# Who issues the weight loads: all of them moved from SyncE's queue to GpSimd's own

## What is computed

```python
x = attention(q, k, v)        # 4 images, 8 heads, 576 positions, head size 64;
                              # mask: block of 64 queries sees its own and earlier blocks of 64 keys
x = transpose(x) -> (2304, 512)
h = x @ moe_w_in              # (512, 1024)
solu = h * softmax(h)
ln = (solu - mean) / sqrt(var + 1e-6) * g_ln
x = ln @ moe_w_out            # (1024, 512)
h = x @ moe2_w_in             # (512, 2048)
g = h * tanh(softplus(h))     # Mish
out = g @ moe2_w_out          # (2048, 512)
```

## Time and profile before

| | us |
|---|---|
| median of 3 runs | 710.01 |
| lowest, highest | 707.37, 711.13 |
| the profiled execution | 708.7 |
| its span | 706.7 |
| PE busy | 691.3 |
| DVE busy | 391.8 |
| ACT busy | 385.0 |
| POOL busy | 82.5 |

### The profile page before, as it was taken

The page is one execution under the profiler, slowest core; times in us unless marked ns, Lnnn a source line. Parts: engine busy times, 40 slices in busy tenths (PEclk is TensorE's granted clock), DMA queues, the critical chain, the costliest instruction groups (busy, mean ns, idle before and its releaser), DMA issues.

```text
span 706.7 us, 15716 instructions
## 1 busy us (share of the span) xinstructions
PE 691.3 (98%) x6490; PEld 465.0 (66%) x6490; DVE 391.8 (55%) x865; ACT 385.0 (54%) x824; POOL 82.5 (12%) x109
## 2 busy tenths in 40 slices
PE   8889999979999999999999999999999999999998
PEld 8558864558547864776468646784588457855873
DVE  6898787773575438543743586627543663352120
ACT  5677875456575555365555664646465554452230
POOL 3121027331000000320000000320000000000000
PEclk9999999999999999999999999999999999999999
DMA  9589875943066506531353176521524164023000
GB/s 273 116 199 212 239 190 134 201 94 58 27 120 127 109 9 117 100 94 45 65 80 77 30 139 130 124 72 29 114 46 61 22 134 91 3 39 74 17 16 30
DMA packets 158518, 68.12 MB, mean 96 GB/s; under 512 B 144368, under 2 KB 147952, under 8 KB 158448
## 3 DMA queue, kind: packets, MB, share of 16 engines
q1 hardware_dynamic: 158448, 67.13, 44.2%
HBM read 26.74 MB, written 4.72 MB: 45 GB/s over the span
## 4 chain that ended last, share of the span: by engine, by line
PE 81%; DVE 7%; ACT 5%; DMA 4%; issue 2%; SPq 0%; ACTq 0%; DVEq 0%
PE banks L805 24%; PE banks L824 24%; PE banks L787 12%; PE banks L774 11%; PE banks L753 4%; PE banks L726 4%; DMA pT<-halves 2%; DVE halves L903 2%; PE banks L715 1%; ACT prob L1054 1%; ACT WH L1078 1%; DVE nmax L890 1%; ACT halves L1062 1%; DMA q_raw<-q 1%; DMA lnT<-ln_split 1%
## 5 line engine op out<-in xcount | busy, mean ns | idle before, releaser
L805 PE MATMUL banks<-x2T_hi,WH 128*128 128x256 f16 x576 | 157.8, 274 | 0.5 <-DVE x2T_lo L974 0.4
L805 PE MATMUL banks<-x2T_lo,WH 128*128 128x256 f16 x576 | 157.8, 274 | 0.0
L805 PE MATMUL banks<-x2T_hi,WL 128*128 128x256 f16 x576 | 157.7, 274 | 0.0
L1054 ACT ACTIVATE prob<-banks,nmax 128x64 f32<-128x64 f32 (+8 forms) x144 | 74.9, 523 | 75.4 <-DVE nmax L890 44.9
L824 PE MATMUL banks<-WH,gT_hi 128*128 128x512 f16 x288 | 109.4, 380 | 0.0
L824 PE MATMUL banks<-WH,gT_lo 128*128 128x512 f16 x288 | 109.2, 379 | 0.0
L824 PE MATMUL banks<-WL,gT_hi 128*128 128x512 f16 x288 | 109.2, 379 | 0.0
L903 DVE SCALAR_TENSOR_TENSOR halves<-prob,rinv,halves 128x64 f16<-128x64 f32 (+8 forms) x144 | 86.7, 616 | 38.3 <-ACT halves L1062 38.1
L983 DVE SCALAR_TENSOR_TENSOR gT_lo<-gbuf,gT_hi 128x512 f16<-128x512 f32 x72 | 50.1, 706 | 101.6 <-ACT gT_hi L1134 101.2
L1062 ACT ACTIVATE halves<-prob,rinv 128x64 f16<-128x64 f32 (+8 forms) x144 | 75.7, 554 | 51.0 <-DVE rinv L898 32.8
L787 PE MATMUL banks<-lnT,WH 128*128 128x256 f16 x576 | 95.9, 273 | 0.0
(11 more groups left out here) (94 smaller groups left out, 997.2 us busy)
## 6 DMA issues: line engine op xcount, KB each, us to landing
w_raw<-w SPq DMA_DIRECT2D x12, 512.0 KB, 5.2
out<-osb SPq DMA_DIRECT2D x18, 256.0 KB, 2.8
q_raw<-q SPq DMA_DIRECT2D x16, 256.0 KB, 3.6
k_raw<-k SPq DMA_DIRECT2D x12, 288.0 KB, 3.5
ln_raw<-w SPq DMA_DIRECT2D x6, 512.0 KB, 4.1
v_raw<-va SPq DMA_DIRECT2D x12, 256.0 KB, 2.7
own_raw<-w SPq DMA_DIRECT2D x4, 512.0 KB, 5.4
pT<-halves SPq DMA_TRANSPOSE x80, 3.7
```

Of the source, the lines that this page charges most:

```text
L805: mm = pe.matmul(banks[:, MI_BANK[n % 2], G * j:G * (j + 1)], w2i(b, c, m), (x2T_hi, x2T_lo)[a][:, c], start=(c == 0 and i == 0), stop=(c ...
L1054: act.activation(prob[:, at:at + width(blk)], scores[:, at:at + width(blk)], ACT.Exp, bias=nmax[:, u % 2, i:i + 1], scale=1.0, accum_out=r ...
```

## The change

All 24 weight loads move from SP's program to POOL's, with the waits ahead of them. POOL issues the first five right after it has built the identity, and the other 19 at their places in `PLAN`. Loads of q, k, v and g_ln, the transposes and the stores stay on SP, in the same order. The amounts, the buffers and the semaphores that count the landings stay as they are.

```diff
@@ block.sync
             def load_w(piece):
                 room, n = room_of(piece)
-                if n > 1:
-                    wait_split(sp, ROOMS[room][n - 2])
-                elif 4 <= room < 6:
-                    sp.wait_ge(ln_lo, TPG)
-                elif 6 <= room < 8:
-                    sp.wait_ge(x2_done, 2)
                 sp.dma_start(raw_of(piece), w[piece]).then_inc(w_in[room], 16)
...
             load_q(0)
             load_first(k_first_raw, k, 1, k_first_in)
             load_first(v_first_raw, va, 0, v_first_in)
-            load_w(0)
             load_first(v_first_raw, va, 1, v_first_in)
-            load_w(1)
             load_q(1)
-            load_w(2)
-            load_w(3)
             sp.dma_start(gsc[:], g_ln).then_inc(g_in, 16)
-            load_w(4)
             load_k(0)
...
-                if kind == "load_w" and of[0] >= 5:
-                    load_w(*of)
@@ block.gpsimd
+            def load_later(piece):
+                room, n = room_of(piece)
+                if n > 1:
+                    wait_split(pool, ROOMS[room][n - 2])
+                elif 4 <= room < 6:
+                    pool.wait_ge(ln_lo, TPG)
+                elif 6 <= room < 8:
+                    pool.wait_ge(x2_done, 2)
+                pool.dma_start(raw_of(piece), w[piece]).then_inc(w_in[room], 16)
...
                                pattern=[[-1, P]], channel_multiplier=1).then_inc(const_pool, 1)
+            for piece in range(5):
+                load_later(piece)
             pool.wait_ge(const_pool, 2)
             pool.wait_ge(const_dve, 1)
             for kind, *of in PLAN:
...
                 if kind == "w2_split":
                     w2_split(*of)
+                if kind == "load_w" and of[0] >= 5:
+                    load_later(*of)
```

## The result

The changed kernel takes 730.7 us (median of 4 runs, 727.53 to 733.62), the kernel before on the same chip 709.92 (4 runs, 707.37 to 711.13). The ratio is 1.030, interval 1.027 to 1.034: **21 us slower**, where 7.6 were forecast. The profiled execution took 727.53 us. In it line 753 of before is L754 (values), 726 is L727 (scores), 824 is L825, 833 is L834; POOL's lines are 13 lower (3 in the splits of 20 to 23).

The account below looks back on a forecast made before the run. TensorE, busy 98% of the span, was taken as the bound; terms 1.3 + 0.6 + 4.0 + 1.7 = 7.6 us on the profiled 708.7 gave 716.3, forecast as 717.6 us for the median, range 712.0 to 724.6.

Parts of the forecast that it names:

- Place 3: Last three loads, 101 to 110 us: two landings lie bare on GpSimd between its splits, TensorE stalls 2L - 4.0, +4.0 us.
- L: Time from issue to landing of a weight load on GpSimd's queue, taken as 4.0 us, bounds 3.6 and 5.9.
- The clock: After TensorE's 4.0 us standstill at the last pieces, matmuls run partly at half clock: +1.7 us, bounds 0 and 1.7.
- Place 1: The start: one more weight served ahead of the second query tile delays TensorE, +1.3 us, bounds 0 and 3.8.
- the first keys and queries leave before it: At the start: first keys and queries leave before GpSimd's first weight load, so one more weight ahead, +1.3 us.
- Place 2: 58 to 60 us: weights 8 and 9 no longer stand behind the transpose of lnT, +0.6 us, bounds 0 and 2.5.
- Other moved issues cost nothing: Weights 5 to 19: each issue costs GpSimd some 0.5 to 1 us, covered by its other work; no term in the sum.
- Weights crowd out the start: Rival: all five weights served before the second query tile, +3.8, both loads hurt lnT, +2.5; 722.0 us, chance 0.18.
- Slow queue: Rival: transfers from GpSimd take over 6 us, stall above 8 us; 721.6 us and more, chance 0.05.
- Short landing: Rival: L is 3.0 us, stall 2.0, no clock loss, no cost at the start or lnT; 712.0 us, chance 0.12.
- Faster: Rival: SyncE's queue, freed of weights, removes TensorE's 4.3 us of idle time before 60 us; 705.7 us, chance 0.05.

Follow-up runs that it names:

- the probe run: Kernel before plus seven dead loads of weight piece 0 from 210 us on, issued by GpSimd, SyncE or ScalarE, all weights on SyncE; one execution, 708.7 us.
- e: Kernel before with pieces 0 to 4 on GpSimd, piece 0 gated on the second keys, 1 to 4 on the second query tile; 710.95 us, ratio 1.0033.
- d: Kernel before with pieces 0 to 4 issued by ScalarE ahead of its table load, all others by SyncE; 712.87 us, ratio 1.0059.
- a: Kernel before with only pieces 0 to 4 issued by GpSimd, the other 19 by SyncE; 713.26 us, ratio 1.0044.
- f: Kernel before with pieces 5 to 19 on GpSimd, load 7 placed later and loads 10 to 12 moved back in the plan; 714.46 us, ratio 1.0089.
- c: Kernel before with only pieces 20 to 23 issued by GpSimd; median 716.0 us, ratio 1.0092.

## Why the prediction was wrong

**Place 3, the last pieces: right in mechanism, near in size, partly by luck.** Forecast a stall of 2L - 4.0 = 4.0 us with L = 4.0. Loads 20 to 23 landed in 3.8, 4.3, 4.8 and 5.4 us; the lag of PE rose by 4.1 us from 108.7 to 121.99, of which the wait for piece 23 is 2.9 and one for a transpose 1.0. Split 20 ended 15.3 us later than before, at 118.75 us, and 118.0 + 4.3 + 4.8 + 15.3 = 142.4 is the end of split 23 to 0.2 us (the memset's 0.3 hides under load 22's landing; without it 142.1). PE was 17.3 us late by then, 2 us more than POOL, so the stall came out 2.9 and not 5.1: landings longer than forecast and a later PE partly cancelled, and the 1.0 us for a transpose, which was not in the sum, brought the rise back to the forecast 4. The sentence that delays of places 1 and 2 carry both engines along and therefore add was only nearly right; with the last four alone, PE was 3.4 us late for another reason and the stall was 0.3 us. By the Trainium skill (DMA: Bandwidth & Descriptors, Anatomy of one DMA), L would have been 3.2 us, an estimate; the trace has 3.8 to 5.4.

**The clock: right as a kind of cost, wrong in place and count.** No loss behind place 3: the granted clock from 142.3 to 146.3 us is 1.00. It fell elsewhere, behind waits that were not forecast (1.9 us before 19.52, 1.9 before 61.07 and 4.7 before 86.49 us). The windows of after that show it:

```profile
19.50:26.50 7.00, 6.98 (x62) 6.03 (x62) 6.43 (x16) 2.90 (x10) 2.25 (x2) 0.76 0.24 56
60.00:66.00 6.00, 4.93 (x61) 4.28 (x62) 5.43 (x11) 3.67 (x8) 1.02 (x1) 0.72 0.38 70
84.00:88.00 4.00, 1.51 (x24) 1.15 (x28) 0.00 (x0) 0.94 (x3) 2.98 (x5) 0.75 0.71 127
```

Length times one less the clock gives 1.7, 1.7 and 1.0 us; 0.7 more follow from 88 to 92 us (clock 0.83). That is 5.1 us, and PE is busy 5.8 us longer, against a forecast of 1.7. Not every such loss is the change's: the probe run, the same as the kernel before up to 210 us, has one from 29 to 34 us, where the kernel before has 1.00 behind the same wait of 1.70 us:

```profile
29.00:34.00 5.00, 4.09 (x31) 1.63 (x32) 4.04 (x14) 3.55 (x13) 0.00 (x0) 0.66 0.53 101
```

So one loss of 1.7 us more or less is scatter between executions, and which of the changed kernel's losses each wait brought is not shown. That they are more is: the mean granted clock of its four executions is 0.986 to 0.991, that of the 29 executions of the kernel before beside the last group 0.993 to 1.00, 0.998 in the mean. Over the span that is 8.6 us lost (0.0118 x 729) against 1.6, so some 7 of the 21 us are the clock's.

**Place 1, the start: term 1.3, bounds 0 and 3.8. Mis-sized, and by more than q1.** The lag is 4.7 us at the score (4.6 with the first five alone). The 1.6 us that bring it to 6 by 20 us are the clock's of the first window above. Median against median the five loads cost 4.6 us, by the ratio 3.1. The working looked at q1 alone, and took one more weight ahead of it. The engines served it among all five: it landed at 16.10 us instead of 12.02, 4.1 us later, just over the bound of 3.8. And two transfers were left out. The second keys, issued at 1.75 us, 0.1 us behind POOL's first load, landed at 9.56 us instead of 6.22; VectorE waited for them, and PE was 2.7 us late at the score that follows:

```profile
9.58 0.43 DVE L857 TENSOR_SCALAR k_hi<-solu 128x512 f16<-128x512 f32 x1 [3.82 <-DMA solu<-k]
```

So "the first keys and queries leave before it" was not enough; leaving first is not landing first. The first part of v, which POOL needs ahead of q_lo, landed at 12.72 us, 10.5 after its issue (4.7 before), the second at 15.47. POOL's first half of v began at 12.92 instead of 7.12 us, and q_lo of this tile, ready to be made from 16.7 us on, stood behind both halves until 18.31.

One thing here is scatter. The first score starts at 6.63 us before and at 8.15 in the changed kernel, because the 25 dummies from 3.3 us on took 4.93 us instead of 3.42: they run 0.21 us apart at first and 0.11 later, and the step comes at 7.5 us instead of 4.4. With 5 to 19, 10 to 12 or 13 to 19 moved nothing differs up to there, and the first score stands at 8.1 to 8.2 us too; in the other traces it stands at 6.7 to 7.4, apart from e (8.15) and d (9.02, with a wait of its own). It adds nothing at the score of the earlier trace rows: a starts its first score at 6.89 us and is as late there.

**Place 2, 58 to 60 us: term 0.6. The step that failed.** I priced lnT alone, and lnT was in fact not hurt in the changed kernel (4.4 us), where POOL's load left 2.3 us behind it. Where it left 1.0 to 1.2 us behind, with 5 to 19 alone and in f, lnT took 6.3 and 5.8 us and PE waited 1.5 and 0.95 us for it: that mechanism exists, at a price within its bounds. From 60 to 80 us I costed "at nothing", with the argument that the transpose of 72.07 us is read only at 97 us. That transpose was the wrong transfer. The v rows issued at 64.36 us have their user at 72.08 us, with 1.6 us of slack, and on SP's queue they and the transpose of 60.81 us stood ahead of weights 10 to 12 (64.88 us and later). In the changed kernel POOL issues 10 and 11 at 70.92 and 71.45 us, ahead of v's rows at 71.56 and 72.63. The transpose took 12.7 us and the v rows 12.2; the v rows came last (84.84 against 80.54 us), and the lag rose from 9.7 to 14.4 us by that one instruction.

**"Other moved issues cost nothing": wrong.** I priced them as issue time on POOL, where they do cost 0.54 to 0.6 us each and hide. What they cost is the transfers beside which they now fly: load 7 at 28 us, 8 to 12 at 60 to 75. 5 to 19 bring 10.4 us against a term of 0.6 for place 2 and nothing for the rest.

**The rivals.** "Weights crowd out the start" had the mechanism, that two queues share the transfer engines, and stayed at 722.0 because it applied it at two places and at the price of the bytes. The Trainium skill (DMA: Bandwidth & Descriptors, Queues, rings and completion order) has each transfer engine take turns between queues; q1 landing together with the weights agrees with that, but the extra 1.7 us of engine time for 512 KB (2.9 less 1.27) are not in it. "Slow queue" is refuted as a property of GpSimd: a load of POOL in a quiet stretch lands in 4.0 us, the last four in at most 5.4, and ScalarE's queue does the same harm at the start. "Short landing" is refuted by L. "Faster" was not seen at any place. The range ended at 724.6, since its upper end priced places 1 and 2 by the bytes and the other loads at nothing; it also took 1.3 for place 2, whose own bound was 2.5, and 725.8 would have missed as well.

**Left open.** Why a mix of packets costs the engines more than the two apart is measured (2.9 against 1.0 us), not explained. That several loads together cost more than their parts is shown, and so is the slack of 1.6 us at 72 us; how much of the rest is the transfers and how much is POOL's program, shifted against VectorE's and ScalarE's, is not separated. And c's profile is of its shortest run, 710.75 us against a median of 716.0, so of its 6.5 us the trace shows only the first 2 to 4.

## What to carry to other kernels

A single queue does two things: it issues, and it keeps an urgent transfer ahead of the bulk that is issued after it. Moving bulk loads to a second queue saves the first engine half a microsecond of issue per load and gives away that order; before it, list every transfer that is in flight with the moved ones and the slack of its reader, since each of these may take two or three times as long (here 7.5 us for 3.5, 12.7 for 7.4, 12.2 for 4.5). A gate in the new engine's program gave the order back here only by holding that engine's own work. And when parts of a change are tried one by one, their sum says little where they share the transfer engines and each delay has a slack to use up first: here three parts that held all the pieces gave 5.4 us and the whole 10.4.

## What the hardware did that I had not expected

A 512 KB load and a transpose that leave together on two queues both slow down: the transpose from 4.3 to 7.5 us with a load that lands in 4.0 (ScalarE's queue), from 3.0 to 3.5 to 7.5 with one that takes 7.2 (GpSimd's). The load adds 2.9 us of transfer time in the first case, and 1.0 ahead of the transpose on the same queue. A load that left 3 us earlier or 2.5 us later did next to no harm, seen once each. Five loads beside one transpose made it take 14.0 us (7.4 before). And the moment at which TensorE's dummies go from 0.21 to 0.11 us apart moved between 4.4 and 7.6 us from one execution to another, with the same program up to there.
